# A fused kernel of gated linear attention and two feed-forward layers: the masked product of k and q reads a narrow copy of q's transposes, in later slots, and the inverse is dealt out over other slots

## The reference

```python
k_n = k / (norm(k) + 1e-6)
for t in range(S):                       # 768 positions
    y[:, :, t] = q[:, :, t] @ state      # read first
    state += beta_t * outer(k_n_t, v_t - state^T k_n_t)
x = y.transpose(0, 2, 1, 3).reshape(3072, 384)
h = x @ w_in                             # 384 -> 2048
x = maximum(0.01 * h, h) @ w_out         # 2048 -> 384
# for rows with x @ w_skip > 0: e = argmax(x @ w_gate),
# out = x + softmax weight * (relu(x @ w1[e]) @ w2[e]), else out = x
```

## Time and profile before

| | |
|---|---|
| median of 3 runs | 895.24 us (892.25 to 895.81) |
| profiled execution's own time | 895.62 us, 0.38 above the median |
| its span, first to last instruction | 893.9 us |
| outside the span | 1.7 us |
| busy: PE, PEld, DVE, ACT, POOL | 774.3, 624.0, 663.7, 495.5, 416.3 us |
| mean granted TensorE clock | 0.976 |

### The profile page before, as it was taken

The page is one execution under the profiler, slowest core; times in us unless marked ns, Lnnn a source line. Parts: engine busy times, 40 slices in busy tenths (PEclk is TensorE's granted clock), DMA queues, the critical chain, the costliest instruction groups (busy, mean ns, idle before and its releaser), DMA issues.

```text
span 893.9 us, 27698 instructions
## 1 busy us (share of the span) xinstructions
PE 774.3 (87%) x10782; PEld 624.0 (70%) x10783; DVE 663.7 (74%) x1334; ACT 495.5 (55%) x1108; POOL 416.3 (47%) x498
## 2 busy tenths in 40 slices
PE   0123679999999999999999999999999899999985
PEld 0123558787777777777778788878777668778764
DVE  6485978888888888788888887866868873563382
ACT  5435555767576766666675766554464652441261
POOL 5213163627262635445453634352353665564473
PEclk9996599999999999999999999999999999999998
DMA  9489748577778777766768676347516765263100
GB/s 224 107 196 194 137 75 140 103 141 139 138 142 139 137 124 133 139 126 131 135 121 145 103 140 123 76 70 232 176 20 205 248 234 182 84 204 118 44 17 17
DMA packets 357277, 119.76 MB, mean 134 GB/s; under 512 B 330450, under 2 KB 348420, under 8 KB 356784
## 3 DMA queue, kind: packets, MB, share of 16 engines
q1 hardware_dynamic: 351424, 104.33, 55.9%
q0 software_dynamic: 3232, 7.64, 2.5%
q10 hardware_dynamic: 2512, 6.29, 2.0%
HBM read 63.53 MB, written 21.25 MB: 95 GB/s over the span
## 4 chain that ended last, share of the span: by engine, by line
PE 32%; DVE 24%; issue 11%; DMA 11%; ACT 11%; SPq 6%; POOL 4%; DVEq 0%; POOLq 0%; ACTq 0%
PE b_acc L849 8%; PE b_h L836 6%; PE b_h L743 6%; PE b_acc L756 6%; DVE stage L1485 4%; SPq L498 4%; DVE inv L1411 3%; DMA t_dram<-inv 3%; PE b_ch L682 3%; DVE inv L1417 3%; DMA natq<-x_dram,id_in 3%; ACT ga L954 2%; DMA operands<-t_dram 2%; ACT operands L954 2%; ACT stage L1074 2%
## 5 line engine op out<-in xcount | busy, mean ns | idle before, releaser
L1910 POOL TENSOR_TENSOR stage<-stage 128x256 f16<-128x256 f32 x192 | 142.7, 743 | 252.9 <-ACT stage L954 252.1
L743 PE MATMUL b_h<-stage,wt 128*128 128x256 f16 x1728 | 221.7, 274 | 11.2 <-DVE stage L1344 9.1
L756 PE MATMUL b_acc<-wt,stage 128*128 128x384 f16 x1152 | 218.4, 326 | 4.3 <-POOL stage L1910 3.4
L743 PEld LDWEIGHTS b_h<-stage,wt 128*128 128x128 f16 x1728 | 158.9, 98 | 31.6 <-DVE stage L1344 10.9
L756 PEld LDWEIGHTS b_acc<-wt,stage 128*128 128x128 f16 x1152 | 106.7, 97 | 59.1 <-POOL stage L1910 6.6
L954 ACT ACTIVATE stage<-stage 128x256 f16<-128x256 f32 x192 | 80.0, 417 | 106.4 <-DVE stage L1485 105.5
L1485 DVE SCALAR_TENSOR_TENSOR stage<-b_h,stage 128x256 f32<-128x256 f32 x192 | 80.8, 421 | 43.2 <-ACT stage L1074 41.6
L849 PE MATMUL b_acc<-wt,operands 128*128 128x384 f16 x552 | 97.3, 326 | 7.6 <-DVE operands L1525 7.6
L836 PEld LDWEIGHTS b_h<-y,wt 128*128 128x128 f16 x1656 | 93.5, 98 | 6.6 <-issue 4.7
L836 PE MATMUL b_h<-y,wt 128*128 128x128 f16 x1656 | 96.5, 219 | 1.6 <-DVE y L1344 0.7
L1417 DVE TENSOR_REDUCE inv<-inv 128x30 f32<-128x90 f32 (+4 forms) x180 | 85.1, 473 | 5.8
(11 more groups left out here) (215 smaller groups left out, 1292.9 us busy)
## 6 DMA issues: line engine op xcount, KB each, us to landing
operands<-in_moe_w_dram SPq DMA_DIRECT2D x18, 1536.0 KB, 7.5
a_sys<-a_dram SPq DMA_DIRECT2D x24, 256.0 KB, 4.3
kc<-operands SPq DMA_DIRECT2D x22, 256.0 KB, 4.1
natq<-in_q_dram SPq DMA_DIRECT2D x24, 192.0 KB, 3.9
raw_v<-in_v_dram SPq DMA_DIRECT2D x24, 192.0 KB, 4.2
stage<-y SPq DMA_DIRECT2D x96, 48.0 KB, 2.0
x_dram<-stage SPq DMA_DIRECT2D x24, 192.0 KB, 2.9
out_dram<-stage SPq DMA_DIRECT2D x24, 192.0 KB, 3.3
```

The costliest lines, as they stand in the source:

```text
L743: mm = pe.matmul(b_h[f % 2][:, 0:GT], wt[0][:, a, d * FF + f * P:d * FF + (f + 1) * P], xT[:, g % 2, b, d, :], start=(i == 0), stop=(i == ...
L756: mm = pe.matmul(b_acc[w][:, 0:DM], g16[:, f % 4, a, w * P:(w + 1) * P], wt[1][:, b, f * DM:(f + 1) * DM], start=(f == 0 and (a, b) == PAR ...
L1910: pool.tensor_tensor(g16[:, f % 4, LO, :], g32[:, f % 4, :], g16[:, f % 4, HI, :], ALU.subtract).then_inc(g_lo, 1)
```

## The change

- A new step compact_q copies the diagonal blocks of qT (64 of 128 columns a unit) into the buffer kc on VectorE, once kT's copy there has been used: two copies of 64 partitions x 2048 f16, in slots 10 and 11, one a slot. gram_p now reads qTc (the same buffer): 64 columns a matmul instead of 128.
- gram_p is two steps of eight units instead of four of four, in slots 13 and 14 (before 10 to 13). VectorE masks twice instead of four times (slots 13, 14), each step with its own pm buffer. p_high and p_low are still four, now each of 64 partitions x 512 (one half of the pair each), since pT is block diagonal now and its other blocks stay at the zeros that GpSimd writes once in the prologue. p_high: slots 14 and 15; p_low: slot 15 and slots 0, 1 of the next turn.
- SHARE: the inverse gets 1 and 2 steps in slots 14 and 15 (before 0 and 1) and ends in slot 10 (before 11); inverse_high and inverse_low move to slot 11 (not in turn 0). seed moves from slot 14 to 13.
- On SyncE inverse_out stands ahead of blocks_back (not in turn 0).
- Waits follow: compact_k waits for gram_p of two groups before, compact_q for q's transposes and for gram_a. GpSimd's constants for the routing move from turn 10 (slots 7 to 10) to turn 11 (slots 0 to 3).

```diff
...
+qTc = kTc
...
-SHARE = (0, 2, 4, 0, 4, 2, 3, 1, 4, 3, 5, 4, 0, 0, 0, 1)
+SHARE = (0, 2, 4, 1, 4, 3, 3, 2, 4, 4, 3, 0, 0, 0, 1, 2)
...
         sp.wait_ge(ga_done, B * g)
+        if g >= 2:
+            sp.wait_ge(gp_done, 2 * (g - 1))
...
             load_k(g + 4)
-        if is_group(g + 2):
+        if g == 0:
+            blocks_back(2)
+        if is_group(g + 1):
+            inverse_out(g + 1)
+        if is_group(g + 2) and g:
...
         if is_group(g + 1):
-            inverse_out(g + 1)
...
 def _(pe):
-    def gram(rhs, g, st):
-        n = rhs.shape[3]
-        for p in range(PAIRS):
-            u = st * PAIRS + p
+    def gram(bank, rhs, g, u0, u1):
+        for u in range(u0, u1):
             for a, b in PARTS:
-                mm = pe.matmul(b_gram[st % 2][:, p * n:(p + 1) * n], kT[g % 2][:, a, u, :], rhs[:, b, u, :],
-                               start=(p == 0 and (a, b) == PARTS[0]), stop=True, skip_group_check=True)
+                mm = pe.matmul(bank[:, (u - u0) * C:(u - u0 + 1) * C], kT[g % 2][:, a, u, :], rhs[:, b, u, :],
+                               start=(u == u0 and (a, b) == PARTS[0]), stop=True, skip_group_check=True)
...
         elif g:
-            pe.wait_ge(pm_ready, B * (g - 2) + 3)
-        gram(kTc, g, st).then_inc(ga_done, 1)
-    def gram_p(g, st):
-        pe.wait_ge(q_turned, 32 * g + 32)
-        if st >= 2:
-            pe.wait_ge(pm_ready, B * g + st - 1)
-        elif is_group(g + 1):
-            pe.wait_ge(ga_ready, B * (g + 1) + st + 3)
-        elif st == 1:
+            pe.wait_ge(pm_ready, 2 * (g - 2) + 1)
+        gram(b_gram[st % 2], kTc, g, st * PAIRS, (st + 1) * PAIRS).then_inc(ga_done, 1)
+    def gram_p(g, s):
+        pe.wait_ge(qc_copied, 2 * g + 2)
+        if is_group(g + 1):
+            pe.wait_ge(ga_ready, B * (g + 1) + s + 3)
+        elif s == 1:
...
             pe.wait_ge(gate_ready, TT * (g - 3) + TT)
-        gram(qT, g, st).then_inc(gp_done, 1)
+        gram(b_gram[s], qTc, g, s * 2 * PAIRS, (s + 1) * 2 * PAIRS).then_inc(gp_done, 1)
...
                 scans[f](g, 0)
-            if nxt and f == 12:
-                gram_p(g + 1, 2 if g else 1)
+            if nxt and f in (13, 14):
+                gram_p(g + 1, f - 13)
...
                 gram_a(g + 2, f - 6)
-            if nxt and f in ((10, 11, 13) if g else (11, 13, 14)):
-                gram_p(g + 1, f - (10 if g else 11))
...
-    def p_high(g, st):
-        act.wait_ge(pm_ready, B * g + st + 1)
-        if g:
-            act.wait_ge(y_done, 2 * g)
-        copy(units(pT, HI, st), pm[st % 2][:]).then_inc(p_hi, 1)
+    def p_high(g, s, x):
+        if x == 0:
+            act.wait_ge(pm_ready, 2 * g + s + 1)
+            if g:
+                act.wait_ge(y_done, 2 * g)
+            else:
+                act.wait_ge(const_pool, 3)
+        h, u = slice(C * x, C * x + C), slice(s * 2 * PAIRS, (s + 1) * 2 * PAIRS)
+        copy(pT[h, HI, u, C * x:C * x + C], pm[s][h].rearrange("p (u c) -> p u c", c=C)).then_inc(p_hi, 1)
...
                 gram_out(g + 2, f - 7)
-            if nxt and f == 12:
+            if nxt and f == (11 if g else 12):
                 inverse_high(g + 1)
-            if nxt and 12 <= f < (15 if g else 16):
-                p_high(g + 1, f - (11 if g else 12))
+            if nxt and f >= 14:
+                p_high(g + 1, f - 14, 0)
...
                 hidden(*up_at(g, f))
-            if nxt and f == 11 and g:
-                p_high(g + 1, 0)
+            if nxt and f >= 14:
+                p_high(g + 1, f - 14, 1)
...
-    def gram_p(g, st):
-        if B * g + st >= 2:
-            dve.wait_ge(p_ready, B * g + st - 1)
-        dve.wait_ge(gp_done, B * g + st + 1)
-        dve.tensor_tensor(pm[st % 2][:], b_gram[st % 2][:], mask_p[:], ALU.mult).then_inc(pm_ready, 1)
+    def compact_q(g, x):
+        if x == 0:
+            dve.wait_ge(q_turned, 32 * g + 32)
+            dve.wait_ge(ga_done, min(B * (g + 2), B * G))
+        h = slice(C * x, C * x + C)
+        dve.tensor_copy(qTc[h], qT[h, :, :, h]).then_inc(qc_copied, 1)
+    def gram_p(g, s):
+        if g:
+            dve.wait_ge(p_ready, B * (g - 1) + 2 * s + 2)
+        dve.wait_ge(gp_done, 2 * g + s + 1)
+        dve.tensor_tensor(pm[s][:], b_gram[s][:], mask_p[:], ALU.mult).then_inc(pm_ready, 1)
...
                 scan_z(g, 0)
-            if nxt and (11 if g else 12) <= f < (15 if g else 16):
-                gram_p(g + 1, f - (11 if g else 12))
+            if nxt and f in (13, 14):
+                gram_p(g + 1, f - 13)
...
                 inverse(n, at, mid)
-            if nxt and f == 12:
+            if nxt and f == (11 if g else 12):
...
                 leaky(*up_at(g, f))
+            if nxt and f in (10, 11):
+                compact_q(g + 1, f - 10)
...
-    def p_low(g, st):
-        pool.wait_ge(p_hi, B * g + st + 1)
-        u = slice(st * PAIRS, (st + 1) * PAIRS)
-        pool.tensor_tensor(pT[:, LO, u, :].rearrange("p u i -> p (u i)"), pm[st % 2][:],
-                           pT[:, HI, u, :].rearrange("p u i -> p (u i)"), ALU.subtract).then_inc(p_ready, 1)
+    def p_low(g, s, x, before):
+        pool.wait_ge(p_hi, B * g + 2 * s + x + 1)
+        if before:
+            pool.wait_ge(g_lo, FT * before[0] + before[1] + 1)
+        h, u, c = slice(C * x, C * x + C), slice(s * 2 * PAIRS, (s + 1) * 2 * PAIRS), slice(C * x, C * x + C)
+        pool.tensor_tensor(pT[h, LO, u, c], pm[s][h].rearrange("p (u c) -> p u c", c=C), pT[h, HI, u, c],
+                           ALU.subtract).then_inc(p_ready, 1)
+        pool.wait_ge(p_ready, B * g + 2 * s + x + 1)
...
                 s_low(g, f - 6)
-            if nxt and (11 if g else 12) <= f < (15 if g else 16):
-                p_low(g + 1, f - (11 if g else 12))
+            if nxt and f == 15:
+                p_low(g + 1, 0, 0, up_at(g, f - 1))
...
                 hidden_low(*up_at(g, f))
-            if g == G - 2 and 7 <= f < 11:
-                constants(f - 7)
+            if nxt and f == 15:
+                p_low(g + 1, 0, 1, up_at(g, f))
+            if scan and g and f < 2:
+                p_low(g, 1, f, up_at(g, f))
+            if g == G - 1 and f < 4:
+                constants(f)
...
     pool.sem_inc(const_pool, 1)
+    link(pool.memset(pT.bitcast(F32), 0.0))
+    pool.sem_inc(const_pool, 1)
...
         kn_low(2, x, None)
-    for st in range(B):
-        p_low(0, st)
+    for s in range(2):
+        for x in range(2):
+            p_low(0, s, x, None)
...
```

43 lines of the change are left out of this document (24 added, 19 removed).

## The result

| | before | after |
|---|---|---|
| median of the runs (us) | 895.52 (892.25 to 896.93, 4 runs) | 928.59 (927.31 to 930.75, 4 runs) |
| span of the profiled execution (us) | 893.9 | 927.4 |
| mean granted clock | 0.976 | 0.978 |

The changed kernel is slower: ratio 1.038, with an interval of 1.035 to 1.041. The forecast was 890.2 us, and its range ended at 902.

A forecast was written before the change was run, and what follows sets the result against it. The prediction took PE to set the time, with short stalls for t_dram and x_low. Turns +0.7, turns 9 and 10 -2.3, prologue and turn 0 -3.4 made -5.0 from 895.6; median 0.4 lower, 890.2 us, range 877 to 902.

The forecast's parts named there:

- Weight loads: Rival on PE's gram_p: weight loads set the pace, 64 columns gain nothing, 896 us; chance 0.03.
- They move: p_high and p_low in later slots: the move costs 0, with -0.5 to +0.6 us a turn.
- Stretch A: From up of slot 10 to scan_u, 21.5 us: falls by 1.4 us in turns 2 to 8.
- the 1.25 us step in slot 15: Inverse step on DVE, put by the new SHARE ahead of leaky and z's first LO half.
- Stretch B: From up of slot 2 to up of slot 10, 24.8 us: grows by 1.5 us, stall from 0.6 to about 2.
- Copies and masks: DVE, slot 10 to slot 0: two copies added, two masks gone, about +0.3 us a turn (0.0 to +2.7).
- The gram's 1.28 us: PE's narrow gram_p: 1.28 us less a group, at most 14.1 us over eleven groups.
- Turns 9 and 10: Turns without a norm or PE gaps: 2 x -1.28 us, less 0.3 for z16, together -2.3 us.
- Prologue and turn 0: Ahead of turn 1: earlier scan_u half and w_out split, shorter inverse_low, masks not waiting: -3.4 us (-6 to +3).
- x_low becomes the bound: slower: Rival on DVE, leaky of slot 4 to x_low in slot 9: 1.9 us of steps, 902 us; chance 0.20.

The follow-up runs named there:

- e5: The kernel before with SyncE's new order alone (inverse_out ahead of blocks_back): 890.40 us, ratio 0.9957.
- e11: e5 without GpSimd's p_low subtraction in its old slots 11 to 14, so that part of the result is missing: 887.58 us, ratio 0.9897.
- e1: The changed kernel with the old SHARE and with inverse_high and inverse_low back in slot 12: 906.67 us, ratio 1.0127.
- e6: e1 without GpSimd's p_low subtraction, so that part of the result is missing: 892.61 us, ratio 0.9981.
- e2: The changed kernel without GpSimd's p_low subtraction, all waits and counts kept: 911.43 us, ratio 1.0181.
- e7: e1 with both copies in slot 10, grams in slots 11 and 12, masks and p_high in 12 and 13, p_low in 13 and 14: 908.16 us.
- e12: e5 with the inverse begun sooner: one step in slot 14, two in 15, two fewer in 10 and 11, seed in slot 13: 904.50 us.
- e10: e3 with one step of the inverse dealt from slot 8 to slot 7: 906.66 us, ratio 1.0107.
- e3: The kernel before with the new SHARE, inverse_high and inverse_low in slot 11, seed in slot 13 and SyncE's new order: 921.48 us, ratio 1.0308.
- e14: e6 without the two copies of q's transposes a turn, so p is wrong: 877.01 us, ratio 0.9787.
- e15: e1 with the copies from group 1 on made by SyncE's DMA queue instead of VectorE: 893.10 us, ratio 0.9968.
- e17: e7 with the copies made by DMA instead of VectorE: 917.47 us, ratio 1.0266.

## Why the prediction was wrong

What held: blocks of 24 products in 0.70 us (222.16 to 222.86 in the changed kernel), copies at 0.68 us, the wait for t_dram gone, a wait for z's low part in its place, turn 10 shorter by 0.9 (1.28 forecast), scan_u's second half in the prologue at about 72 us instead of 75.65 (its products follow the first half's without a gap from 71.00 on). Weight loads don't set the pace.

The steps that failed, with what they measured:

*"They move ... I book the move at 0, with -0.5 to +0.6 us a turn."* This was the largest error in kind. p_low costs 3 us (5) in all in slots 11 to 14 and 14 us (13) in slots 15, 0 and 1 (e5, e11, e1, e6), 17 in the changed kernel (e2): about +1.5 us a turn. I had the row that shows it, the copy of 2.02 us beside GpSimd, and applied it to the copies, which ran undisturbed here: by luck, for the first of them starts 0.13 us before kn_low's end, and e7's second copy, in another place, was held. It fits just as well the operations that read two operands from SBUF, z's low part and the inverse's products, and for these I didn't ask. I looked at what is moved and not at what it is moved beside.

*Stretch A, -1.4 us.* It grew. In turn 5 it runs from 367.56 to 389.43, 21.9 us against 21.5. The earlier start of the inverse costs 14 us (12) by itself (e12), 0.9 us a turn. I named the 1.25 us step in slot 15 and set against it the slack of 1.3 us that the next sentence gave to PE's earlier arrival; and the step took 1.49 us, with a second one of 128 x 512 behind it.

*Stretch B, +1.5 us, stall 2 us.* The stall was 2.34 us; from scan_u to up of slot 10 turn 5 has 29.4 us (338.17 to 367.56) against 27.0 (322.60 to 349.64), +2.4. Its cause was mostly another one. I counted steps; e10 has the same count ahead of x_low's second half as e3 and lacks the collision with nat_k, and it is 15 us faster. The deal shifted the order of products and reductions against nat_k, and a product of 0.38 us became one of 1.37. On e3's stall of 2.35 us, 0.7 are there anyway, the steps that I priced at 1.5 us a turn (0.7 to 1.9) bring 0.6 (e10 against e12), and the collision 1.0. So DVE absorbs more than half of the steps, and that the stall came out nearly as forecast was luck: its larger part had a cause that I hadn't seen.

*Copies and masks, "about +0.3 us a turn", absorbed by 7.7 idle us.* The copies had the price that I gave them, 0.68 each, but the idle time covers nothing in slots 10 to 12: 1.3 us a turn (e14, and e15 by DMA). The two masks that go gave nothing back that I can show. The gram's 1.28 us came through as 0.7 (e14) and 1.17 (turn 9) where the copies or the norm of k were missing, and as a loss of 0.6 where both were there (e11, e6). The gram's part of the change is therefore worth +5 us (+7.5), not -14.

*Turns 9 and 10, -2.3 us.* +1.1 and -0.9. Turn 9 still has p_low beside z.

*Prologue and turn 0, -3.4 us.* In turn 0 the up of slot 10 stands at 104.96 against 105.50, -0.5, and by the first scan product of turn 1 it is +0.7. scan_u's second half did come some 3.6 us sooner, but the next thing in line is DVE's share of w_out's split, which waits for ACT and now lies beside p_low, stretched from 1.76 to 2.55 us:

```profile
75.87 2.55 DVE L1352 SCALAR_TENSOR_TENSOR wt<-stage,wt 128x1536 f16<-128x1536 f32 x1 [4.61 <-ACT wt L957]
...
79.27 1.12 PE L687 MATMUL b_ch<-u,operands 128*128 128x48 f16 x24 [6.16 <-DVE u L1457]
```

The rival "x_low becomes the bound: slower", at 902, had the right sign and place, but with steps for its price. It left out z, which was the greater half: PE waits there 21.3 us.

The prices by part, from runs that each undo or do one: SyncE's order -5 (-4), the narrow gram without p_low +5 (+7.5), p_low's new slots +11 (+8; 14 less the 3 of the old ones, 13 less 5), the deal on top of these +22. They sum to the 33 measured, but as differences along one way from the kernel before to the changed one they must, so the sum is no proof of them. On another way the prices differ: on the kernel before alone the deal costs 31 us (30) (e3 against e5). That its own wait for z and p_low's are in part the same 1 to 2 us would explain it; no run tested that.

Still open: what takes the remaining 0.6 us of the gram's 1.28 in turns 2 to 8, what part the seed's new slot has in the gate's wait, and why some stalls of 2.3 us are followed by the lower clock and others not. e17 joins SyncE's order, the copies by DMA and an early p_low, and loses: with kc shared, the copy must follow k's last gram in slot 9.

## What to carry to other kernels

Before an operation of GpSimd is moved, or a list of VectorE's steps is shifted by one, lay the two timelines side by side and mark which of VectorE's operations read two operands from SBUF (and f16 copies like those here): each of them that starts well inside a GpSimd operation ends behind it. One such meeting ahead of a critical wait cost 1.0 us a turn here, and some 15 us in all with the lower clock behind the longer stall. Give those places to reductions and to operations with an input in PSUM. An engine's idle time per turn is no cushion: it covers added work only in the slots where it lies, so price an added operation in full if the slot before the next critical wait is unbroken. And when a change has several parts, time the smallest one alone: here a swap of two lines in a DMA queue was the only part with a gain.

## What the runs showed of the hardware

- A VectorE TENSOR_TENSOR with two SBUF inputs that starts inside a GpSimd operation ends at GpSimd's end plus its own undisturbed length less 0.14 us. z's low part ends 0.42 us behind (0.56 alone, 1.11 held), the product of 128 x 220 0.24 us (0.38 alone, 1.37 held), L1418 0.55 us (0.69 alone, 1.33 held). In the traces of the 19 kernels, from 130 to 640 us, and with the median of the same form in the same kernel as the undisturbed length, this holds within 0.03 us for 776 of 777 such operations that started at least 0.2 us before the end of a GpSimd TENSOR_TENSOR. So a meeting costs what GpSimd's operation still has to run, less 0.14 us, and nothing if that is 0.13 us (the first copy of the changed kernel).
- The copies of 64 x 2048 f16, with one input, follow the same rule: e7's second one, 0.64 us before GpSimd's end, takes 1.19 us instead of 0.68.
- A tensor_reduce (0.56 us) and an operation with one of its two inputs in PSUM (0.55 us) were not delayed beside nat_k. The same holds for 106 TENSOR_TENSORs with an input in PSUM that started inside a GpSimd operation: none was off its usual length by more than 0.02 us.
- Behind a stall of 2.3 us PE's granted clock was 0.54 for 3.7 us in some turns, and the 15 matmuls of one up and one down took 3.6 instead of 1.95 us; in other turns the same stall left it at 1.00.
- 24 products of 64 columns, each with its weight load, take 0.70 us, 29 ns apiece (the changed kernel).
- A copy within SBUF in two DMAs of 256 KB each costs SyncE 1.7 to 3.9 us of issue and VectorE nothing, and each lands 3.2 to 5.9 us after its issue, 4.1 at the median (e15); the same copy on VectorE takes 1.37 us in two operations.
